# Experts' weights in spaced pieces, zero products ahead of the first keys, and a reordered start

## What is computed

```python
for t in range(S):                      # attention by a delta rule, 32 heads, 768 steps
    y[:, :, t] = np.einsum('bhd,bhde->bhe', q[:, :, t], state)
    v_old = np.einsum('bhde,bhd->bhe', state, kt)
    state = state + bt[:, :, :, None] * np.einsum('bhd,bhe->bhde', kt, vt - v_old)
...
d = exp(logits - logits.max(0)); d /= d.sum(0)       # soft mixture: 8 experts, 4 slots each
h = np.maximum(slot_input[e] @ w1[e], 0.0); slot_out[e] = h @ w2[e]
x = softmax(logits, 1) @ slot_out
...
h = x @ w_in; out = (h * sigmoid(1.702 * h)) @ w_out  # 3072 x 384, 2048 inner
```

## Time and profile before

| | us |
|---|---|
| median of 3 runs | 534.46 |
| the runs | 533.6 to 537.81 |
| the profiled execution, its own time | 532.87 |
| its span, first to last instruction | 531.1 |

### The profile page before, as it was taken

One profiled execution on the slowest core, in us unless ns is written; L12 is line 12 of the kernel. 1 busy time (PEld: TensorE's weight loads), 2 busy tenths in 40 slices (PEclk: granted clock), 3 DMA queues, 4 the chain that ended last, 5 costly groups with the idle time before them and its releaser, 6 DMA issues.

```text
span 531.1 us, 17585 instructions
## 1 busy us (share of the span) xinstructions
PE 457.2 (86%) x7288; PEld 338.8 (64%) x7288; DVE 355.8 (67%) x1182; ACT 309.4 (58%) x704; POOL 8.2 (2%) x20
## 2 busy tenths in 40 slices
PE   5647788787787778869999789999999999999997
PEld 4433566656555456655544268778888888888885
DVE  3797979889999878434562367666566566566563
ACT  2212668878878788855522256565655655655653
POOL 2000000000000000000000000000000000000000
PEclk9999879999999889998999989999999999999999
DMA  8601264634222124394499800010000100100101
GB/s 326 254 1 55 74 245 128 246 128 141 90 88 64 47 84 155 88 413 159 169 400 410 330 0 1 0 60 0 31 29 0 59 0 0 59 0 0 61 0 60
DMA packets 23367, 59.18 MB, mean 111 GB/s; under 512 B 2176, under 2 KB 10368, under 8 KB 22912
## 3 DMA queue, kind: packets, MB, share of 16 engines
q1 hardware_dynamic: 23296, 58.15, 30.4%
HBM read 53.43 MB, written 4.72 MB: 109 GB/s over the span
## 4 chain that ended last, share of the span: by engine, by line
PE 60%; ACT 18%; DVE 10%; issue 8%; DMA 3%; ACTq 0%; DVEq 0%
PE bank L786 11%; PE bank L788 10%; PE bank L787 10%; ACT zb L798 9%; PE bank L502 8%; PE bank L764 3%; ACT nv L841 3%; PE bank L451 3%; PE bank L488 3%; PE bank L643 2%; ACT state L798 2%; DVE g_l L1286 2%; DVE g L1283 2%; DMA wo<-in_w_out 2%; ACT g_h L798 2%
## 5 line engine op out<-in xcount | busy, mean ns | idle before, releaser
L786 PE MATMUL bank<-g_h,wo_h 128*128 128x512 f32 x288 | 113.2, 393 | 2.7 <-DVE g_l L1286 2.5
L1286 DVE TENSOR_TENSOR g_l<-g,g_h 128x512 fp32r<-128x512 f32 x96 | 66.5, 693 | 72.1 <-ACT g_h L798 72.1
L787 PE MATMUL bank<-g_h,wo_l 128*128 128x512 f32 x288 | 112.6, 391 | 0.0
L788 PE MATMUL bank<-g_l,wo_h 128*128 128x512 f32 x288 | 112.6, 391 | 0.0
L798 ACT ACTIVATE g_h<-g 128x512 fp32r<-128x512 f32 x96 | 60.7, 633 | 77.9 <-DVE g L1283 77.9
L1081 DVE TENSOR_TENSOR tt<-tt,tmp 128x110 f32<-128x110 f32 (+35 forms) x366 | 76.1, 252 | 0.2
L1076 DVE TENSOR_TENSOR tmp<-nm,tt 128x110 f32<-128x110 f32 (+35 forms) x366 | 75.7, 251 | 0.3
L1283 DVE TENSOR_TENSOR g<-bank,sig 128x512 f32<-128x512 f32 x96 | 66.2, 690 | 10.9 <-ACT sig L965 6.2
L502 PE MATMUL bank<-zb,kn 128*32 128x192 f32 (+1 forms) x736 | 43.1, 349 | 33.1 <-ACT zb L798 30.9
L798 ACT ACTIVATE state<-bank 48x384 f32<-48x384 f32 x92 | 44.7, 485 | 39.0 <-PE bank L502 38.1
L798 ACT ACTIVATE zb<-bank 32x192 f32<-32x192 f32 x192 | 61.7, 321 | 8.3 <-PE bank L488 5.9
(11 more groups left out here) (144 smaller groups left out, 443.1 us busy)
## 6 DMA issues: line engine op xcount, KB each, us to landing
kq<-in_kq_t SPq DMA_DIRECT2D x24, 512.0 KB, 5.4
slice<-in_w SPq DMA_DIRECT2D x6, 2048.0 KB, 10.0
slice<-in_w SPq DMA_DIRECT2D x8, 1536.0 KB, 13.6
vn<-in_v_nat SPq DMA_DIRECT2D x24, 192.0 KB, 3.9
out_t<-res SPq DMA_DIRECT2D x18, 256.0 KB, 2.0
kn<-in_k_nat SPq DMA_DIRECT2D x23, 192.0 KB, 2.5
win<-in_w_in SPq DMA_DIRECT2D x3, 1024.0 KB, 16.8
wo<-in_w_out SPq DMA_DIRECT2D x4, 768.0 KB, 11.7
```

Source lines behind the costliest of these rows:

```text
L786: eng.matmul(acc[d][:], wo_h[:, f, cols], g_h[:, f % GR], start=(f == 0), stop=False)
L787: eng.matmul(acc[d][:], wo_l[:, f, cols], g_h[:, f % GR], start=False, stop=False)
L788: i = eng.matmul(acc[d][:], wo_h[:, f, cols], g_l[:, f % GR], start=False, stop=(f == NF - 1))
L1286: eng.tensor_tensor(g_l[:, f % GR], g[:, f % GR], g_h[:, f % GR].bitcast(F32), ALU.subtract).then_inc(s_gl, 1)
```

## The change

1. **Transfers.** Slices 0 and 1 are asked for one expert (512 KB) at a time at chunks 4 to 11, behind the chunk's second `solve`; slice 3 one expert at a time at chunks 16 to 19; slices 2, 4, 5 and 6 in 32 pieces of half an expert (64 partitions), eight to a chunk in chunks 20 to 23, each behind a wait for another step of the chunk. The rest of the slices are asked for where they were, in four transfers each. The values of chunk c + 3 are asked for behind its natural keys. The keys of chunks 4 to 9 wait for the third `gram`.
2. **Start on PE.** A tile of zeros is filled first on DVE, and five products on it (384 columns) stand ahead of the first `gram`. `ks(0, 0)` stands ahead of the later warm-up, which has four products.
3. **Start on DVE.** `squares(0)` stands ahead of the fourth mask. `scale_v(0)` and `right_side(0, 0)` stand four elimination steps before the end. In `scales` the small transpose stands behind the large product.
4. **Turns.** One turn at chunk 14, three at 15 to 20, two at 21, one at 22, two at 23 (`TURN_AT`). The Exp table is loaded at chunk 20. The first maximum covers the groups 0 to 4.

```diff
+TURN_AT = {NCH - 10: (None, None, 0), NCH - 9: (1, 2, 3), NCH - 8: (4, 5, 6), NCH - 7: (7, 8, 9), NCH - 6: (10, 11, 12),
+           NCH - 5: (13, 14, 15), NCH - 4: (16, 17, 18), NCH - 3: (19, 20, None), NCH - 2: (21, None, None),
+           NCH - 1: (22, None, 23)}
-GCA = CA // 4
+GCA = 5
...
+def loads_of(i):
+    return EG * DMA * (2 if i in (2, 4, 5, 6) else 1)
...
+            def load_expert(i, q):
+                eng.dma_start(w_slices[i][:, q], weights_of(i, q)).then_inc(s_w[i], DMA)
+
+            def load_expert_half(i, q, h):
+                rows = slice(64 * h, 64 * h + 64)
+                eng.dma_start(w_slices[i][rows, q], weights_of(i, q)[rows]).then_inc(s_w[i], DMA)
+
             def load_slice(i):
-                eng.dma_start(w_slices[i][:], src).then_inc(s_w[i], DMA)
+                for q in range(EG):
+                    load_expert(i, q)
...
             eng.dma_start(beta[:], beta_m).then_inc(s_beta, DMA)
+            eng.wait_ge(p_g, CR - 1)
             for c in range(CR, GA):
                 load_kq(c)
...
+            late = [(i, q, h) for i in (2, 4, 5, 6) for q in range(EG) for h in range(2)]
             for c in range(NCH):
-                if c in (2, 5):
-                    load_slice(c // 3)
                 if c + QR < NCH:
                     eng.wait_ge(p_q, c + 1)
                     load_kq(c + QR)
+                if CR <= c < 3 * CR:
+                    eng.wait_ge(p_z, 2 * c + 2)
+                    load_expert((c - CR) // EG, (c - CR) % EG)
+                if NCH - 2 * CR <= c < NCH - CR:
+                    eng.wait_ge(p_q, c + 1)
+                    load_expert(3, c % EG)
+                if c >= NCH - CR:
+                    if c == NCH - CR:
+                        eng.wait_ge(v_d, NR)
+                    places = ((p_z, 2 * c + 1), (p_k, 2 * c + 2), (p_q, c + 1), (p_s, min(2 * c + 1, 2 * LAST)), (p_z, 2 * c + 2),
+                              (p_k, min(2 * c + 3, 2 * NCH)), (p_s, min(2 * c + 2, 2 * LAST)), (p_y, c + 1))
+                    for n, (done, count) in enumerate(places):
+                        eng.wait_ge(done, count)
+                        load_expert_half(*late[2 * CR * (c - NCH + CR) + n])
+                if c + 3 < LAST:
+                    eng.wait_ge(p_s, 2 * c + 2)
+                    load_kn(c + 3)
                 if c + 3 < NCH:
                     eng.wait_ge(v_nv, c + 1)
                     eng.wait_ge(a_nv, c + 1)
                     load_vn(c + 3)
...
# PE
+            eng.wait_ge(z_rr, 1)
+            zeros = rr[:].rearrange("p g e -> p (g e)")
+            for _ in range(5):
+                eng.matmul(rz[1][:, 0:NG * D], zeros[:, 0:P], zeros[:], start=True, stop=True)
             for c in range(GA):
                 for a in range(2):
                     gram(c, a)
-
-            eng.wait_ge(v_c, WARM_AT)
-            warm_up(5)
             eng.wait_ge(z_s, 3)
             ks(0, 0)
+            eng.wait_ge(v_c, WARM_AT)
+            warm_up(4)
...
-            slots(3, yp[0], False, True).then_inc(p_sa, 1)
+            slots(3, yp[0], False, False).then_inc(p_sa, 1)
+            slots(4, yp[0], False, True).then_inc(p_sa, 1)
...
# ACT
-                if c == FIRST:
-                    eng.activation(one["tab"][:, 0:1], mask[:, 0:1], ACT.Exp).then_inc(s_table, 1)
...
+                if c == NCH - CR:
+                    eng.activation(one["tab"][:, 0:1], mask[:, 0:1], ACT.Exp).then_inc(s_table, 1)
...
# DVE
+            eng.memset(rr[:], 0.0).then_inc(z_rr, 1)
             for t in (state, *sp):
                 eng.memset(t[:], 0.0).then_inc(z_s, 1)
             eng.memset(zb[:], 0.0).then_inc(z_zb, 1)
-            for c in range(CR):
+            for c in range(CR - 1):
                 masked(c)
             squares(0)
+            masked(CR - 1)
             masked(CR)
             scales(0)
             for j in range(C - 1):
                 eliminate(0, j)
                 if j in MASKED_AT:
                     masked(MASKED_AT[j])
-            scale_v(0)
-            right_side(0, 0)
+                if j == C - 6:
+                    scale_v(0)
+                    right_side(0, 0)
             inverted(0)
```

More of the change, by code:

```diff
@@ L436, in warm_up @@
                 for _ in range(n):
-                    eng.matmul(rz[0][:], data[:, 0:P], data[:, P:P + 512], start=True, stop=True)
+                    eng.matmul(rz[1][:], data[:, 0:P], data[:, P:P + 512], start=True, stop=True)
             def gram(c, a):
@@ L549, in turn, with e_turned @@
                 i.then_inc(p_xt, 1)
-            def e_turned(phase, bank, src):
+            def e_turned(phase):
                 eng.wait_ge(a_e, phase + 1)
-                for j, part in enumerate(src):
-                    i = eng.transpose(bank[:, P * j:P * j + P], part, ident[:])
+                for group in ((0, 1, 2, 3, 4), (5,))[phase]:
+                    src = e_parts[:, 0:P] if phase else lgt[:, group]
+                    i = eng.transpose(sp[group // 4][:, P * (group % 4):P * (group % 4) + P], src, ident[:])
                 i.then_inc(p_e, 1)
@@ L572, in _ @@
                     gram(c, a)
-            eng.wait_ge(v_c, WARM_AT)
-            warm_up(5)
             eng.wait_ge(z_s, 3)
             ks(0, 0)
+            eng.wait_ge(v_c, WARM_AT)
+            warm_up(4)
             for c in range(NCH):
-                ahead, late = c + GA < NCH, TURNS * (c - FIRST)
+                ahead, turns = c + GA < NCH, TURN_AT.get(c, NO_TURNS)
                 solve(c, 0)
@@ L585, in _ @@
                 else:
-                    e_turned(0, sp[0], [lgt[:, i] for i in range(GCA)])
+                    e_turned(0)
                 if ahead:
                     gram(c + GA, 0)
-                if late >= 0:
-                    turn(late)
+                if turns[0] is not None:
+                    turn(turns[0])
                 solve(c, 1)
@@ L595, in _ @@
                     gram(c + GA, 1)
-                if late >= 0:
-                    turn(late + 1)
+                if turns[1] is not None:
+                    turn(turns[1])
                 if c < LAST:
@@ L607, in _ @@
                     slots(1, yp[0], False, False)
-                if late >= 0:
-                    turn(late + 2)
+                if turns[2] is not None:
+                    turn(turns[2])
             slots(2, yp[0], False, False)
             logits_of(NGT - 1)
-            slots(3, yp[0], False, True).then_inc(p_sa, 1)
+            slots(3, yp[0], False, False).then_inc(p_sa, 1)
+            slots(4, yp[0], False, True).then_inc(p_sa, 1)
             by_tokens(NGT - 1)
-            e_turned(1, sp[1], [e_parts[:, P * j:P * j + P] for j in range(NGT - GCA)])
+            e_turned(1)
             eng.wait_ge(v_diag, 1)
@@ L865, in _ @@
             eng.wait_ge(z_s, 1)
-            eng.activation(rr[:, 0, 0:1], state[:, 0, 0, 0, 0:1], ACT.Sqrt).then_inc(s_table, 1)
+            eng.activation(one["tab"][:, 0:1], state[:, 0, 0, 0, 0:1], ACT.Sqrt).then_inc(s_table, 1)
             eng.wait_ge(s_table, 1)
@@ L876, in _ @@
             for c in range(NCH):
-                r, late = c // CR + 1, TURNS * (c - FIRST)
-                mine = late >= 0 and c < NCH - CR
+                r, turns = c // CR + 1, TURN_AT.get(c, NO_TURNS) if c < NCH - CR else NO_TURNS
                 z_out(c, 0)
@@ L901, in _ @@
                     scale_v(c + 1)
-                if mine:
-                    turn_out(eng, copy, late + 2)
+                if turns[2] is not None:
+                    turn_out(eng, copy, turns[2])
+                if c == NCH - CR:
+                    eng.activation(one["tab"][:, 0:1], mask[:, 0:1], ACT.Exp).then_inc(s_table, 1)
                 if c == LAST - 1:
@@ L1148, in _ @@
             for c in range(NCH):
-                r, steps, late = c // CR + 1, ELIMINATE[c % CR], TURNS * (c - FIRST)
-                mine = c >= NCH - CR
+                r, steps, turns = c // CR + 1, ELIMINATE[c % CR], TURN_AT[c] if c >= NCH - CR else NO_TURNS
                 right_side(c, 1)
@@ L1153, in _ @@
                     slot_max(0)
-                if mine:
-                    turn_out(eng, eng.tensor_copy, late)
+                if turns[0] is not None:
+                    turn_out(eng, eng.tensor_copy, turns[0])
                 if c == 0:
@@ L1167, in _ @@
                     masked(c - 1 + GA)
-                if mine:
-                    turn_out(eng, eng.tensor_copy, late + 1)
+                if turns[1] is not None:
+                    turn_out(eng, eng.tensor_copy, turns[1])
                 if c == NCH - CR:
@@ L1180, in _ @@
                     c_shift(0)
-                if mine:
-                    turn_out(eng, eng.tensor_copy, late + 2)
+                if turns[2] is not None:
+                    turn_out(eng, eng.tensor_copy, turns[2])
                 if r < NR:
```

64 lines of the change are left out of this document (23 added, 41 removed).

## The result

| | median, us | ratio to the kernel before, 95% interval |
|---|---|---|
| before | 535.10 | |
| changed | 527.71 (526.62 to 528.09) | 0.9853 [0.9809, 0.9897] |
| changed, measured again later | 528.89 (526.69 to 529.97) | 0.9873 [0.9836, 0.9911] |

The changed kernel is 1.3 to 1.5% faster: 7.4 us by the first medians, 6.4 by the second. The forecast was 526.5 us, by a gain of 8.1. The two profiled executions lie only 5.6 us apart (spans 531.1 and 525.5).

The account below looks back on a forecast made before the run. Bound by the PE and ACT chain in the chunks, with code stops behind weights, then by transfers. +0.4 - 2.0 - 9.2 + 1.5 + 0.7 + 0.5 = -8.1 from the median 534.46: 526.5 us, range 520 to 532.5.

Parts of the forecast that it names:

- The start: Before the chunks: later keys of chunk 4 cost +0.4 us, the inverse's earlier begin on DVE gains 2.0.
- the 2.0 us claimed: Start on DVE: removing 2.15 us of idle time ahead of `right_side(0, 0)` and reordering work starts the inverse earlier.
- The delay of `scales(0)`: Start: `scales(0)` waits for the mask of chunk 4, whose keys come later; +0.4 us, between -0.6 and +1.5.
- Stops that go: Chunks 1, 2, 6, 21 and 22: PE's stops for code late behind weights vanish; -9.2 us, lower bound -1.
- Stops that come: Chunks 4 to 11: spaced 512 KB experts sometimes delay code packets; +1.5 us, bounds 0 and 15.
- rival C: Slower: spacing puts a burst into every chunk, all eight from 4 to 11 pay 1.9; 541 us, chance 0.07.
- The 3.5 us from request to use: PE's code in the chunks: about 3.5 us against 4 us of work per block leaves some 0.5 to spare.
- Turns and table: Chunks 14 to 23: moved turns and Exp table load sum to +0.7 us, between -1 and +2.
- the term that I took as 1.5: Added turns: 1.0 us for three at chunk 15 and 0.5 for the one at chunk 14.
- Behind the chunks: Transfer-bound stage before the last layer: last half piece ahead of slice 7 costs +0.5 us; four-way slices cost 0.
- the rate of the half pieces: Chunks 20 to 23: 0.26 MB pieces take 0.65 us each, about the spare time; cost 0, at most 4 times 1.9.
- Round by packet: DMA engines alternate queues packet by packet, so code waits behind at most one weights packet; -9.2 would become 0.

Follow-up runs that it names:

- the square of four kernels: The kernel before and the changed kernel, plus each with the other's weight transfers: old kernel with pieces 532.50 us, changed kernel with whole slices 531.37 us.
- the spacing alone: The kernel before with only the changed weight pieces, places, waits and order of values and natural keys; old start, turns and table load: 532.50 us, ratio 0.9945.
- the kernel with narrow products: The changed kernel with its five zero products narrowed from 384 columns to 16: 527.49 us, ratio 0.9848.

## Why the prediction was right, and where its steps failed

Time, sign and likeliest case came out: 527.7 against 526.5, and the stops in chunks 2 and 6 went with the bursts. But the profiled gain, 5.6, is 2.5 less than the forecast 8.1: the start fell short by 0.9 and the stage behind the chunks by 2.9, against 0.7 more than forecast in the chunks and 0.5 in the last layer. That the medians came within 0.7 us of the forecast gain, and 1.7 in the repeat, is luck in part, by which execution stood for a kernel.

- **The start**: -1.6 forecast, -0.7 measured. The inverse follows `scales(0)` by 25.7 us instead of 27.8, the 2.0 us claimed. The delay of `scales(0)` was +1.4, at the upper end of what I gave (-0.6 to +1.5): the keys landed at 15.9, not 15.2, and their `gram` ran at the low level, 2.25 us. PE's warm-up, 0.81 us a record, never reached the high level. I had taken its last records for fast (an end at 43.7); it ended at 45.97, just ahead of the first `solve` at 46.25, and so cost nothing.
- **Stops that go**: -9.2 forecast. Chunks 1 and 2 together gave -3.6, as forecast, and chunk 6 -1.9. For chunk 2 and chunk 6 the step is shown by the square of four kernels. The 1.7 us in chunk 1, where I gave 1.0 to values that no longer move with the keys, are not the spacing's: with the spacing alone chunk 1 keeps its stop. In chunks 21 and 22 the burst's stops are gone as well, for the -3.7 that I gave, but with pieces a stop stood there or in the last chunk in three other profiles (1.81, 2.64 and 1.21 us), where I had put 0. This part came out, and isn't shown.
- **Stops that come**: +1.5 forecast for chunks 4 to 11, +1.1 measured, in 10 and 11. In the three other profiles with the same code and transfers up to there, chunks 10 and 11 took 2.6, 0.7 and 0.9 us more than before. Two chunks of eight are hit, not all as in rival C. That the pieces are what hits them is not shown: the kernel with narrow products has the same pieces and no such stop. The 3.5 us from request to use that I put in for a packet stands in no view; the rows give 2.8 us from the packet at 100.5 to PE going on.
- **Turns and table**: the three turns of chunk 15 cost 0.1 and the one of chunk 14 nothing; the term that I took as 1.5 was covered (the slow products of chunk 15 in the kernel before, 1.50 us for half an `update`, are fast now). The table's cost moved from chunk 16 to the chunk behind its new place, 21. The last chunk, which should have gained, lost 0.8: turn 22 in its first place waits 1.19 us for y's copy on ACT, a wait that I had not looked for. Against twice 8.84 us, chunks 21 and 22 took +1.2, with the last chunk's +0.8, chunk 16's -1.4 and +0.1 the sum is +0.7, as forecast: right by luck.
- **Behind the chunks**: the step that failed. I gave +0.5 and measured +3.4; from the end of `pz` to the last layer it should have stayed within 1.5 us. The term that was mis-sized is the rate of the half pieces. I took 415 GB/s from a row of whole 128-partition transfers, for pieces of 64 partitions, of which the kernel before has none; they run at 229. 5.5 MB at that rate fill the engines for 24 us of the 35 they have, with the rest of the 7.5 MB until the last chunk's end, and the queue of the next stage starts behind 0.7 MB of them: 2.1 us. The other 1.2 are PE's lower clock behind a longer wait for m, which a new order of two copies on ACT takes away. The rule that I had quoted against it, from the Trainium skill (DMA: Bandwidth & Descriptors, Rules for kernel authors), asks for 128 partitions and at least 1 MiB. The trace agrees with the first half of it (229 against 311 GB/s) and not with the second, for queued transfers: pieces of 384 KB and 128 partitions ran at 400 GB/s from 255 to 280 us.
- **Round by packet**: by the rule on the order of queues in the Trainium skill (DMA: Bandwidth & Descriptors, Queues, rings and completion order), as I had applied it, no stop would have gone. The runs speak against that use of it: chunk 2 is 1.7 to 2.5 us longer with the burst in both pairs, and packets of code 6 us apart were seen under a burst twice (94.5 to 100.5, 91.5 to 97.5). Whether the packet waits in a DMA engine, or is asked for or used late, no run here shows.

## What to carry to other kernels

Where PE stops inside a group that has nothing to wait for, look for its code packets and for what fills the DMA engines then; spread big loads over the time in which the engines idle, and compare several executions, for where a stop falls is partly chance. Try a cut of a load along its columns before one along its partitions (here 311 against 229 GB/s, though the median didn't move), and leave the queue empty where a stage begins that lives on transfers. In a list worked through in order, put nothing that waits for a transfer ahead of a copy that the next products need.

## What the runs showed of the hardware

- Transfers of 64 partitions (4 or 3 KB from each) moved at 229 GB/s with all DMA engines shown 96% busy; the same bytes from 128 partitions (2 or 1.5 KB each) at 311 GB/s. The larger packets were the slower.
- PE stopped for 0.9 to 3.4 us, mostly 1 to 2, in the middle of unconditional work, in every one of the thirteen profiles. Of six bursts of 2 MB (slices 0, 1 and 3, in two kernels) the four in chunks 2 and 6 had a stop and the two at chunk 16 none; with single transfers of 512 KB stops came now and then.
- With the same start code the eight records of the warm-up took 6.52, 6.36, 6.30, 6.13 and 5.78 us in five profiles: how much of it runs at the high level differs from one to the next. In the kernel before the granted clock reads 1.00 from 0 to 45 us though its products are spaced as at 1.2 GHz (0.85 us for 512 columns twice), while in the changed one it reads 0.50 from 15 to 45. The spacing of the products is the better witness.
